# Turning x on VectorE from early block loads, and finding whole turns on ScalarE

## The reference, cut to what matters

```python
# 1. gated linear attention, 4 batches x 8 heads, 768 tokens, head size 48
state = alpha_t[:, None] * state + k_t v_t^T ;  x_t = q_t state
# 2. mixing (x is now 4 x 768 x 384)
theta = x @ w_theta
zr, zi = x * cos(theta), x * sin(theta)
u = x + w_tok_r @ zr + w_tok_i @ zi          # over tokens
u = u + relu(u @ w_ch)
# 3. feed forward, 1024 wide
h = relu(u @ w_in);  c = conv of 3 tokens over h
y = (h * sigmoid(c)) @ w_out
```

## Time and profile before

| | |
|---|---|
| three runs | 531.76, 532.25, 532.94 us; median 532.25 |
| span of the profiled execution | 530.5 us; no device time of that execution stands beside it, so the runs' median is used, 1.75 us above the span |
| busy | PE 522.1, PEld 513.2, DVE 441.2, ACT 287.4, POOL 72.0 us |
| PE transposes of x, L1450 | 72 instructions |
| DMA | 37163 packets, 56.93 MB; 29.3% of 16 engines' span on SP's queue |
| mixing | from about 96 to 317 us of the span |

### The profile page before, as it was taken

One profiled execution on the slowest core, in us unless ns is written; L12 is line 12 of the kernel. 1 busy time (PEld: TensorE's weight loads), 2 busy tenths in 40 slices (PEclk: granted clock), 3 DMA queues, 4 the chain that ended last, 5 costly groups with the idle time before them and its releaser, 6 DMA issues.

```text
span 530.5 us, 11806 instructions
## 1 busy us (share of the span) xinstructions
PE 522.1 (98%) x4142; PEld 513.2 (97%) x4142; DVE 441.2 (83%) x801; ACT 287.4 (54%) x607; POOL 72.0 (14%) x65
## 2 busy tenths in 40 slices
PE   8999999999999999999999999999999999999997
PEld 7999988999999999999999999999999999999997
DVE  8999996997886759767786777999888888889874
ACT  4889887765534434444344542555555454545353
POOL 5988893000000000000000000000000000000000
PEclk9999999999999999999999999999999999999999
DMA  8999987476131020211062011202020110201011
GB/s 326 336 308 361 313 302 224 120 236 222 40 104 31 17 70 25 96 30 54 15 205 94 1 45 56 80 2 90 0 89 30 59 56 33 89 0 47 0 46 44
DMA packets 37163, 56.93 MB, mean 107 GB/s; under 512 B 3328, under 2 KB 27392, under 8 KB 37120
## 3 DMA queue, kind: packets, MB, share of 16 engines
q1 hardware_dynamic: 34000, 51.65, 29.3%
q10 hardware_dynamic: 3120, 4.72, 2.5%
HBM read 42.20 MB, written 14.16 MB: 106 GB/s over the span
## 4 chain that ended last, share of the span: by engine, by line
PE 92%; SPq 2%; DVE 2%; DMA 2%; issue 1%; ACT 0%; POOL 0%; DVEq 0%; ACTq 0%
PE y_bank L1475 26%; PE y_bank L1534 19%; PE theta_bank L1521 10%; PE x_bank L1521 10%; PE y_bank L1505 7%; PE theta_bank L1462 7%; PE weighed L1372 4%; PE x_sum L1330 3%; PE x_sum L1345 2%; PE turned L1357 2%; SPq L734 1%; PE x_bank L1450 1%; DMA x_in<-x_scratch 1%; PE turned L1377 1%; PE x_sum L1316 1%
## 5 line engine op out<-in xcount | busy, mean ns | idle before, releaser
L1534 PE MATMUL y_bank<-first_w,z 128*128 128x384 f32 x576 | 109.5, 335 | 0.0
L1534 PEld LDWEIGHTS y_bank<-first_w,z 128*128 128x128 f32 x576 | 101.2, 188 | 0.0
L1475 PE MATMUL y_bank<-first_w,z 128*128 128x384 f32 x432 | 78.0, 337 | 0.1
L1475 PE MATMUL y_bank<-rest_w,z 128*128 128x384 f32 x432 | 76.9, 336 | 0.0
L1475 PEld LDWEIGHTS y_bank<-first_w,z 128*128 128x128 f32 x432 | 74.5, 188 | 0.3 <-issue 0.3
L1475 PEld LDWEIGHTS y_bank<-rest_w,z 128*128 128x128 f32 x432 | 74.7, 188 | 0.0
L1045 ACT ACTIVATE out_rows<-theta_bank 128x386 f32<-128x386 f32 x32 | 15.8, 493 | 50.6 <-PE theta_bank L1521 50.5
L1275 DVE TENSOR_SCALAR x_rows<-out_rows,taps 128x384 f32<-128x384 f32 x64 | 26.8, 419 | 19.5 <-ACT out_rows L1045 19.4
L1462 PE MATMUL theta_bank<-theta_w,x_t 128*128 128x384 f32 x216 | 41.6, 336 | 0.1
L1278 DVE SCALAR_TENSOR_TENSOR x_rows<-out_rows,taps,x_rows 128x384 f32<-128x384 f32 x64 | 39.6, 619 | 2.3
L1282 DVE SCALAR_TENSOR_TENSOR z_full<-out_rows,taps,x_rows 128x384 f32<-128x384 f32 x64 | 39.6, 619 | 2.2
(11 more groups left out here) (126 smaller groups left out, 974.9 us busy)
## 6 DMA issues: line engine op xcount, KB each, us to landing
a_in<-in_a_rows SPq DMA_DIRECT2D x15, 390.0 KB, 5.8
k_in<-in_k_rows SPq DMA_DIRECT2D x15, 384.0 KB, 5.7
q_in<-in_q_rows SPq DMA_DIRECT2D x14, 384.0 KB, 5.3
v_in<-in_v_tokens SPq DMA_DIRECT2D x16, 288.0 KB, 4.8
x_in<-x_scratch SPq DMA_DIRECT2D x24, 192.0 KB, 2.5
y<-x_all SPq DMA_DIRECT2D x7, 576.0 KB, 3.2
u_scratch<-u_sum ACTq DMA_DIRECT2D x6, 576.0 KB, 3.5
u_first<-u_scratch SPq DMA_DIRECT2D x4, 577.5 KB, 4.4
```

The lines of the kernel that those rows point to most:

```text
L1475: ins = pe.matmul(y_bank[2 * d + half][:, 0:HALF], z[s % 2][part][zp][:, d * P:(d + 1) * P], mixing_w(part, wp, s)[:, half_tokens(half)], ...
L1534: ins = pe.matmul(out_bank[half][t][:, 0:MODEL], g[k % 4][gp][:, t * P:(t + 1) * P], out_w[wp][f], start=f == 0 and i == 0, stop=f == FF_T ...
```

## The change

`turn` and `hold` go. In their place SP loads each tile a second time (`load_blocks`), into a new ring of three buffers x_blocks: four DMAs, one for each 32 tokens, each of 32 features x 12 x 32 tokens, that is 384 runs of 128 bytes. The 32x32 blocks so stand where DVE's block transpose (`flip`, one instruction over 128x384) turns each in its place, and x_tokens comes straight from it. In `angle`, the two instructions L1172 and L1174 move from DVE to ACT (`whole_turns`, two ACTIVATE with Copy).

```diff
@@ pair_step, at i == JUDGED_AT
             do.load_first(2)
+            do.load_blocks(0, 0)
+            do.load_blocks(0, 1)
@@ pair_tail
             do.refill_piece(n)
+        do.load_blocks(0, 2)
         do.halve(0, 0)
...
-        do.turn(0, 0)
         do.lower(0, 0)
         do.theta_low()
         do.theta(0, 0)
-        do.turn(0, 1)
         do.scan_state(p)
         do.low(0)
-        do.hold(0, 0)
+        do.flip(0, 0)
         do.high(1)
         do.halve(0, 1)
-        do.hold(0, 1)
         do.angle(0, 0)
@@ mix_batch
             tile(do.load, b, s + 3, last)
+            tile(do.load_blocks, b, s + 3, last)
+            tile(do.flip, b, s + 1, last)
             if s == T - 1:
                 do.mix(b, s)
                 do.sums(b)
             tile(do.halve, b, s + 2, last)
-            tile(do.hold, b, s + 2, last)
             if not (isinstance(b, int) and b == 0 and s == 0):
                 tile(do.theta, b, s + 1, last)
             tile(do.angle, b, s + 1, last)
             tile(do.sines, b, s + 1, last)
-            tile(do.turn, b, s + 2, last)
             tile(do.lower, b, s + 2, last)
@@ SP
-            for t in (x_turned, x_low, x_kept):
+            for t in (x_low, x_kept):
                 t.before(sp, b * T + s, 3)
             load_tile(b, s)
+
+        def load_blocks(b, s):
+            x_flipped.before(sp, b * T + s, 3)
+            for t in range(P // BLOCK):
+                sp.dma_start(x_blocks[s % 3][t * BLOCK:(t + 1) * BLOCK, :, :],
+                             x_scratch.rearrange("b (n p) t -> b p n t", p=BLOCK)[b, :, :, s * P + t * BLOCK:s * P + (t + 1) * BLOCK]
+                             ).then_inc(blocks_got[s % 3].sem, 16)
@@ ACT, in place of hold
+        def whole_turns(b, s):
+            n = b * T + s
+            theta_made.done(act, n)
+            z_done.before(act, n, 1)
+            act.activation(turns[:, :], theta_bank[:, 0:MODEL], ACT.Copy, bias=ROUND, scale=1 / (2 * np.pi)).then_inc(turned_by.sem, 1)
+            turned_by.done(act, n)
+            act.activation(turns[:, :], turns[:, :], ACT.Copy, bias=-ROUND).then_inc(whole.sem, 1)
@@ DVE, angles
-            z_done.before(dve, n, 1)
-            dve.tensor_scalar(turns[:, :], theta_bank[:, 0:MODEL], 1 / (2 * np.pi), ROUND, ALU.mult, ALU.add).then_inc(turned_by.sem, 1)
-            turned_by.done(dve, n)
-            dve.tensor_scalar(turns[:, :], turns[:, :], ROUND, None, ALU.subtract).then_inc(whole.sem, 1)
             whole.done(dve, n)
@@ DVE
+        def flip(b, s):
+            n = b * T + s
+            blocks_got[s % 3].done(dve, b * (T // 3) + s // 3)
+            z_done.before(dve, n, 2)
+            dve.transpose(x_tokens[s % 2][:, :], x_blocks[s % 3][:, :, :].rearrange("p n t -> p (n t)")).then_inc(x_flipped.sem, 1)
@@ PE: turn is removed
-            for d in range(MODEL_TILES):
-                ins = pe.transpose(x_bank[:, d * P:(d + 1) * P], x_in[s % 3][:, d, :], ident[:, :])
-            ins.then_inc(x_turned.sem, 1)
```

More of the change, by code:

```diff
@@ L24 @@
 HALO = 1
+BLOCK = 32
 WIDE = HALF + 2 * HALO
@@ L223 @@
 PLACES = """refill_piece score scan_after scale_k spread cap by_token inside scan_before scale_q mask mask_late select added
-scan_state high bring keep low theta_high theta_low compare waves refill refill_v judge place divert decide store store_half store_late halve hold turn lower theta angle sines
-product round_z fill load load_first load_weight spare prepare mix sums end send join front gate split back_ff fetch""".split()
+scan_state high bring keep low theta_high theta_low compare waves refill refill_v judge place divert decide store store_half store_late halve flip lower theta angle sines
+product round_z fill load load_first load_blocks load_weight spare prepare mix sums end send join front gate split back_ff fetch""".split()
 Work = namedtuple("Work", PLACES, defaults=[nothing] * len(PLACES))
@@ L469, in layer @@
     x_in = ring("x_in", 3, [P, MODEL_TILES, P])
+    x_blocks = ring("x_blocks", 3, [P, MODEL // BLOCK, BLOCK])
     x_rows = ring("x_rows", 2, [P, SEQ])
@@ L601, in layer @@
     x_got = [tally(f"x_got{i}", 16) for i in range(3)]
-    x_turned, theta_made, mixed = tally("x_turned", 1, 3), tally("theta_made", 1, 1), tally("mixed", 2, 2)
-    x_high, x_low, x_moved, x_kept = tally("x_high"), tally("x_low", 1, 3), tally("x_moved", 1, 1), tally("x_kept", 1, 3)
+    blocks_got = [tally(f"blocks_got{i}", 16 * (P // BLOCK)) for i in range(3)]
+    theta_made, mixed = tally("theta_made", 1, 1), tally("mixed", 2, 2)
+    x_high, x_low, x_flipped, x_kept = tally("x_high"), tally("x_low", 1, 3), tally("x_flipped", 1, 3), tally("x_kept", 1, 3)
     turned_by, whole, first, second, bounded = (tally(x, 1, 1) for x in ("turned", "whole", "first", "second", "bounded"))
@@ L836, in _ @@
         program(sp, Work(refill_piece=refill_piece, refill=refill, refill_v=refill_v, decide=decide, store=store, store_half=store_half, store_late=store_late, load_first=load_first,
-                         load=load, load_weight=load_weight, spare=spare, prepare=prepare, end=store_u, back_ff=back_ff))
+                         load_blocks=load_blocks, load=load, load_weight=load_weight, spare=spare, prepare=prepare, end=store_u, back_ff=back_ff))
         stored[0].done(sp, BATCH - 1)
@@ L979, in halve @@
             act.activation(x_t[0][:, :, :], x_in[s % 3][:, :, :], ACT.Copy).then_inc(x_high.sem, 1)
-        def hold(b, s):
+        def whole_turns(b, s):
             n = b * T + s
-            x_turned.done(act, n)
-            z_done.before(act, n, 2)
-            act.activation(x_tokens[s % 2][:, :], x_bank[:, 0:MODEL], ACT.Copy).then_inc(x_moved.sem, 1)
+            theta_made.done(act, n)
[3 more added lines that the diff above has]
+            act.activation(turns[:, :], turns[:, :], ACT.Copy, bias=-ROUND).then_inc(whole.sem, 1)
         def sines(b, s):
@@ L1073, in _ @@
         act.activation(unused[:, :], state_decay[0][:, 0, ENTERED:], ACT.Copy)
-        for t in (x_moved, sized, sined, cosined, z_high, *u_stored, c_high, h_done, gate_done, g_high, evacuated):
+        for t in (turned_by, whole, sized, sined, cosined, z_high, *u_stored, c_high, h_done, gate_done, g_high, evacuated):
             t.open(act)
@@ L1079, in _ @@
         program(act, Work(by_token=by_token, mask_late=mask_late, keep=keep, spread=spread, cap=cap, high=high, theta_high=theta_high, compare=compare, waves=waves,
-                          halve=halve, hold=hold, sines=sines, round_z=round_z, load_weight=load_weight, spare=spare,
+                          halve=halve, angle=whole_turns, sines=sines, round_z=round_z, load_weight=load_weight, spare=spare,
                           prepare=prepare, sums=sums_of, send=send, fetch=fetch, front=front, gate=gating, split=split, back_ff=back_ff))
@@ L1127, in scan_before @@
             if i == 1:
-                for t in (x_low, turned_by, whole, first, second, bounded, z_done, x_kept, u_done, out_done,
+                for t in (x_low, x_flipped, first, second, bounded, z_done, x_kept, u_done, out_done,
                           c_low, conv1_done, conv2_done, conv3_done, gated_done, z_low, g_low, in_low):
@@ L1188, in product @@
             z_low.before(dve, n, 1)
-            x_moved.done(dve, n)
+            x_flipped.done(dve, n)
             for part, (wave_of, ready) in enumerate(((sine, sined), (cosine, cosined))):
@@ L1307, in _ @@
         program(dve, Work(scan_after=scan_after, scan_before=scan_before, place=place, mask=mask, scan_state=scan_state,
-                          divert=divert, lower=lower, angle=angles, fill=fill, product=product, theta_low=theta_low, low=low, round_z=round_z, load_weight=load_weight, sums=sums_of, end=end, spare=spare,
+                          divert=divert, lower=lower, flip=flip, angle=angles, fill=fill, product=product, theta_low=theta_low, low=low, round_z=round_z, load_weight=load_weight, sums=sums_of, end=end, spare=spare,
                           prepare=prepare, fetch=fetch, front=front, gate=gating, split=split))
@@ L1510, in join @@
         def join():
-            x_moved.done(pe, LAST_TILE)
             first.done(pe, LAST_TILE)
@@ L1536, in back_ff @@
                 ins.then_inc(added_up.sem, 1)
-        for t in (x_turned, theta_made, mixed, multiplied, h_made, added_up):
+        for t in (theta_made, mixed, multiplied, h_made, added_up):
             t.open(pe)
@@ L1545, in _ @@
         pe.wait_ge(dve_const, N_DVE_CONST)
-        program(pe, Work(inside=inside, bring=bring, added=added, judge=judge, score=score, divert=divert, turn=turn, theta=theta,
+        program(pe, Work(inside=inside, bring=bring, added=added, judge=judge, score=score, divert=divert, theta=theta,
                          mix=mix, end=end, join=join, front=front, back_ff=back_ff))
@@ L1591 @@
     from concourse.bass_utils import run_bass_kernel_spmd
-    nc = bacc.Bacc("TRN2", target_bir_lowering=False, num_devices=1)
```

(1 more changed line is left out.)

## The result

| | median (range), runs | profiled span |
|---|---|---|
| before | 532.46 us (531.76 to 532.94), 4 | 530.5 us |
| after | 535.0 us (534.26 to 535.84), 4 | 532.7 us |

The ratio after to before is 1.005, 95% interval 1.0034 to 1.0067: slower by half a per cent. 532.4 had been forecast, with 531.3 to 533.3 for the likeliest case and 528.8 to 537.5 over all cases. The profiled execution of after took 534.49 us, 1.8 above its span. The span grew by 2.2 us. A second set of six runs of the same kernel gave 535.53 us.

What follows compares the result with a forecast made beforehand. PE per tile in the steady part and SP's issue list in batch 0 were taken to bound it; 5.6 us late in batch 0 and 5.6 given back cancel: span 530.5, plus 1.75, said as 532.4 us, range 528.8 to 537.5.

Steps and rivals of the forecast that it cites:

- likeliest case: Whole kernel: the late batch 0 and the later gain cancel, 531.3 to 533.3 us; chance 0.34.
- PE, 5.6 us given back: From batch 0's last mix on: 17 turns still to come go, 0.33 us each, 5.6 us in all.
- Chain from theta to z, flip: Steady part: DVE's first multiply-add 1.55 us after theta's end, flip 0.55 us, both hidden.
- Block loads, DMA engines: Each tile adds 1600 small packets, 17 to 28 ns each, about 2.2 us on 16 engines; hidden.
- Rival 1: DMA engines become the bound in batch 0 from 36 ns a packet; 536.0 us at 45 ns; chance 0.27.
- Block loads, SP: Four more issues per tile at 0.46 us, 1.84 us a tile; hidden in the steady part, not in batch 0.
- The 12 early issues: Block issues for tiles 0 to 2, 5.5 us, ahead of the last stores; hidden by SP's wait for ACT.
- step (a): Start of batch 0: whole turns on ACT move DVE's first multiply-add and PE's first mix 0.5 us later.
- (c): Batch 0, tile 5: whole turns queue behind weight piece 10 on ACT; last mix at 141.5, 5.6 us late.
- its own sign: Batch 0's last mix: the forecast is wrong if it starts before 140 or after 143 us.
- rival 2: SP's delay in batch 0 is smaller, by 3.2 us together, 529.1 us; chance 0.33 with what leads the same way.
- Rival 3: Steady part: the gain is not given back, the period stays at 8.1 us, 537.9 us; chance 0.06.

Runs made afterwards that it cites:

- e4: The kernel after, with the same 16 block-load DMAs of four tiles carrying 3 of 12 feature blocks; 533.75 us, ratio 1.0037 to before.
- e1: The kernel before, with only the whole turns moved to ScalarE, turn and hold kept; 533.65 us, ratio 1.0046.
- e5: The kernel after, unchanged, run again in a second set; 535.53 us, ratio 1.0067 to before.
- e8: The kernel after, with whole turns back on DVE and the blocks of four tiles issued by GpSimd; 526.57 us, ratio 0.9897 to before.
- e9: The kernel after, with the blocks of four tiles issued by GpSimd, whole turns still on ScalarE; 526.29 us, ratio 0.9874 to before.
- e2: The kernel after, with whole turns back on DVE; 534.76 us, ratio 1.0047 to before.
- e10: The kernel after, with whole turns back on DVE, run again in a later set; 533.45 us, ratio 1.0005 to before.
- e7: The kernel after, with turn and hold kept in batch 0, flip and block loads from batch 1 on; 528.98 us, ratio 0.9948 to before.

## Why the prediction came out as it did

The mechanism was right, and the time lies in the range, but the range is wide: it covers three rivals with their own mechanisms. The likeliest case by itself, 531.3 to 533.3, misses the 535.0 by 1.7 us, and the forecast value is 2.6 low. Slower, as measured, had a chance of 0.33 and no change 0.34, so the forecast did not call the sign, and only the wide range holds 535.0. By its steps:

- **PE, 5.6 us given back: 4.9.** The turns went at 0.33 us each. Mis-sized because a turn at the end of a batch covered PE's wait for u_part (0.2 us on the chain in each of three batches); the text asked what hides each added piece, and not what the removed one had been hiding.
- **Chain from theta to z, flip: right in kind.** T + 1.6 to 1.7 for 1.55 in most tiles, 2.25 in the first one shown; 0.57 us for 0.55; both hidden.
- **Block loads, DMA engines: hidden as said, and cheaper.** 38,401 more packets added 34.9% x 532.7 x 16 - 29.3% x 530.5 x 16 = 488 us of engine time, 12.7 ns each, under the lower bound of 17. From 144 to 149 us of after, a tile load and its blocks alone (2000 packets, 39.0% of 5 us on 16 engines, less 400 at 27.7 ns) give 12.6. Rival 1, at 36 ns and more, does not hold. By e4, three quarters of the packets of four tiles are worth 1.8 us or less. The page's rule of 512 bytes at least (the Trainium skill, DMA: Bandwidth & Descriptors, Specifications) is right in its direction, since a byte costs 1.8 times as much (128 bytes in 12.7 ns against 512 in 27.7), and decides nothing here.
- **Block loads, SP: right in kind, 0.46 too low.** A block's issue is followed by the next after 0.51 us, 2.04 us a tile, 16 x 0.05 = 0.8 us over batch 0. Piece 10 was issued at 132.34 (131.6) and took 3.7 us to ACT's start (3.3). The 12 early issues were not quite hidden: in after SP has no pause above 0.4 us from 82 us on, and its last four stores begin at 97.96, though ACT's last copy is done at 96.94.
- **Batch 0, step (a): right for after** (mix 0 at 96.20, +0.5), and only because the flip had removed hold (e1). **(c):** DVE's first multiply-add of tile 5 at 138.33 (137.0), the last mix at 143.02 (141.5), so 7.1 us late and not 5.6. By its own sign, a last mix after 143, the forecast is wrong, by a hair in this profile and clearly in e5 (145.20). What failed is the size of the delay and not its cause: 0.7 from the issues, 0.4 from the landing, and the rest from the chain behind it.

7.1 - 4.9 = 2.2 us of span. The sum had two terms of near 5.6 that cancelled, and both were off in the same direction, by 1.5 and 0.7. The remaining 0.5 us between the profiled run and the median is spread of the runs. In rival 2 the long issue of SP was to fall where SP idles. SP no longer idles there, and long issues stay (1.78 us at 87.79, 1.02 at 98.95 and 1.17 at 125.44 in after): they stand at the same times in every profile and not at the same DMA, so that moving the list does not move them out of it. Rival 3 did not happen.

The rival that the text did not weigh is the one that would have been worth most: SP's list as something that can be put elsewhere. e8 and e9 show that the loss goes when another queue issues 16 of the DMAs.

## What to carry to other kernels

An issuing engine is a resource like the others: where it issues without pause, each DMA added cost about half a microsecond here for all behind it, with 12 KB as with 48, and the same loads cost nothing that could be seen from a queue that was idle. Before you shift work to an engine in order, look at what stands ahead of it in that queue at the tightest place: the same two instructions on ScalarE cost 1.6 or 1.7 us behind hold, and nothing that the medians show in e9. And when you take out work, ask which wait it had been covering.

## What the runs showed of the hardware

- A half-clock stretch followed PE's idle time of 3.48 us (after), 3.42 (e2) and 4.09 (e10). It added 1.4 and 1.6 us to the mix behind it in e2 and e10, 0.4 us for each us of the wait. In e5 a wait of 3.01 us was followed by a stretch at 0.67 (132 to 136 us), and one of 3.04 by none: the mix behind it took its 6.48 us at full clock. None is seen in PEclk of e9 either, where PE's longest wait at the start of batch 0 and in it was 1.42 us. The Trainium skill (TensorE: Matmul & The Clock Gate, Part 1) says that an idle PE falls to 1.2 GHz; these traces agree, but for the second wait of e5. PE's timeline of e5:

```profile
145.20 6.48 PE L1480 MATMUL y_bank<-rest_w,z 128*128 128x384 f32 x36 [3.04 <-DVE z L1213]
```

- GpSimd issued a block load of 384 runs in 0.61 to 0.68 us, SP in 0.47; landing took 3.2 to 3.5 us in place of 2.3 to 2.4. On GpSimd's queue the profile counts one packet for 12 runs, of about 115 ns (59 us for 512), and not 12 of 12.7.
- Single issues of SP of 0.9 to 2.2 us, in place of 0.3 to 0.5, begin at nearly the same times in all twelve profiles, whatever DMA they are of: one between 97.6 and 100.0 us, one between 120.5 and 125.5, in eight of them one more between 87 and 90. What makes them is not shown. The spread of the runs (in e7 528.33 to 533.11) may come from them; that was not tried.
